# Regrouping six turned probability tiles four to two, and reordering the first steps of a tanh feed-forward, in a one-core attention and mixture kernel

## The reference, cut to what matters

```python
def _attn_ref(q, k, v, proj):                 # 2 batches, 8 heads, 768 tokens, 64 wide
    q_bucket, k_bucket = ...                  # from the signs of q @ proj, k @ proj (6 bits)
    scores = where(q_bucket[:, None] == k_bucket[None], (q @ k.T) / 8, -1e9)
    attn = exp(scores - scores.max(-1)); attn /= attn.sum(-1) + 1e-9
    return attn @ v

def _moe_ref(x, phi, w1, w2):                 # x: 1536 x 512, 32 slots, 8 experts of width 1024
    logits = x @ phi
    slot_out = experts(softmax(logits, 0).T @ x)        # 32 x 512
    return softmax(logits, 1) @ slot_out

def _moe2_ref(x, w_in, w_out):                # w_in: 512 x 2048, w_out: 2048 x 512
    h = x @ w_in
    return (h - tanh(h)) @ w_out
```

## Time and profile before

| | |
|---|---|
| median of 3 runs | 498.12 us (497.16 to 500.0) |
| the profiled execution's own time | 497.75 us |
| its span, first to last instruction | 496.0 us |
| mean granted TensorE clock | 0.990 of full |
| busy: PE, DVE, ACT, POOL | 92%, 74%, 68%, 31% |

### The profile page before, as it was taken

The page is one execution under the profiler, slowest core; times in us unless marked ns, Lnnn a source line. Parts: engine busy times, 40 slices in busy tenths (PEclk is TensorE's granted clock), DMA queues, the critical chain, the costliest instruction groups (busy, mean ns, idle before and its releaser), DMA issues.

```text
span 496.0 us, 9754 instructions
## 1 busy us (share of the span) xinstructions
PE 458.6 (92%) x3509; PEld 359.6 (73%) x3509; DVE 368.4 (74%) x779; ACT 339.1 (68%) x666; POOL 153.5 (31%) x198
## 2 busy tenths in 40 slices
PE   1599999999999999999998997987989999999996
PEld 0488888888887988979887341454767888888885
DVE  2478777877778787787886519038969999998992
ACT  3287786877868777786662126047769999999971
POOL 1044241432505325052000100004434555446530
PEclk9999999999999999999999999799999999999999
DMA  8544819357292662615609999980000020001002
GB/s 215 133 99 114 265 43 267 103 129 249 49 300 64 153 231 51 153 33 145 229 4 355 375 386 386 387 314 1 1 1 1 0 85 2 0 32 55 2 1 85
DMA packets 33840, 68.16 MB, mean 137 GB/s; under 512 B 3328, under 2 KB 5504, under 8 KB 33792
## 3 DMA queue, kind: packets, MB, share of 16 engines
q1 hardware_dynamic: 33792, 67.54, 43.5%
HBM read 58.09 MB, written 3.15 MB: 123 GB/s over the span
## 4 chain that ended last, share of the span: by engine, by line
PE 80%; DVE 8%; DMA 8%; issue 1%; SPq 1%; ACT 1%; POOL 0%; DVEq 0%; ACTq 0%
PE b L892 14%; PE b L876 13%; PE b L1054 8%; PE b L865 8%; PE b L1055 8%; PE b L1056 8%; PE b L866 7%; DMA ring_b<-in_w 3%; DMA ring_x<-in_w 3%; PE b L848 3%; PE b L979 2%; PE b L1041 2%; PE b L904 2%; DVE st L627 1%; DMA qk<-bits 1%
## 5 line engine op out<-in xcount | busy, mean ns | idle before, releaser
L627 DVE TENSOR_REDUCE st<-b 128x1 f32<-128x768 f32 x96 | 91.4, 952 | 50.8 <-PE b L866 50.7
L436 ACT ACTIVATE probs<-b,st 128x768 f32<-128x768 f32 x96 | 94.9, 988 | 35.6 <-DVE st L630 34.7
L393 POOL TENSOR_TENSOR uu<-uu,sq 128x256 f32<-128x256 f32 x94 | 74.3, 812 | 121.9 <-ACT uu L499 121.9
L876 PE MATMUL b<-const,probs 128*128 128x128 f32 x576 | 84.0, 277 | 1.0 <-DVE pt L639 0.5
L865 PE MATMUL b<-qk 96*128 96x384 f32 x192 | 75.5, 393 | 5.8 <-DMA qk<-bits 5.8
L1054 PE MATMUL b<-woh,gh 128*128 128x512 f32 x192 | 76.2, 397 | 4.5 <-DVE gl_a L765 3.4
L876 PEld LDWEIGHTS b<-const,probs 128*128 128x128 f32 x576 | 68.8, 142 | 10.1 <-DVE pt L639 5.5
L1055 PE MATMUL b<-wol,gh 128*128 128x512 f32 x192 | 75.2, 392 | 0.0
L892 PE MATMUL b<-pt,vn 128*64 128x128 f32 x1152 | 73.5, 277 | 0.7 <-ACT pt L447 0.7
L892 PEld LDWEIGHTS b<-pt,vn 128*64 128x64 f32 x1152 | 61.9, 137 | 15.1 <-ACT pt L447 9.6
L447 ACT ACTIVATE pt<-b 128x384 f32<-128x384 f32 x96 | 46.7, 487 | 32.1 <-PE b L876 32.1
(11 more groups left out here) (116 smaller groups left out, 709.1 us busy)
## 6 DMA issues: line engine op xcount, KB each, us to landing
ring<-in_w SPq DMA_DIRECT2D x15, 1024.0 KB, 8.4
ring_b<-in_w SPq DMA_DIRECT2D x12, 1024.0 KB, 11.5
raw<-in_k SPq DMA_DIRECT2D x32, 192.0 KB, 3.9
raw<-in_q SPq DMA_DIRECT2D x32, 192.0 KB, 4.3
ring_x<-in_w SPq DMA_DIRECT2D x5, 1024.0 KB, 11.3
wo_raw<-in_w_out SPq DMA_DIRECT2D x1, 4096.0 KB, 14.8
win<-in_w_in SPq DMA_DIRECT2D x4, 1024.0 KB, 14.2
vn<-in_v SPq DMA_DIRECT2D x8, 384.0 KB, 5.1
```

Of the source, the lines that this page charges most:

```text
L393: ins = pool.tensor_tensor(uu[:, r, cols], uu[:, r, cols], sq[:, r, cols], ALU.mult)
L436: act.activation(probs[:, h].rearrange("p (a n) -> p a n", a=2), score[h][:, :].rearrange("p (a n) -> p a n", a=2)[:, :, 0:HALF], ACT.Exp, ...
L627: dve.tensor_reduce(neg, score[h][:, :].rearrange("p (a n) -> p a n", a=2)[:, :, 0:HALF], AX.XY, ALU.max, negate=True).then_inc(max_done, 1)
L876: ins = pe.transpose(ptp[:, a * 512 + t * P:a * 512 + (t + 1) * P], probs[:, h, (3 * a + t) * P:(3 * a + t + 1) * P], ident[:, :])
```

## The change

It has two parts.

**In the attention**, the six turned tiles of a unit are grouped four and two instead of three and three. TensorE writes four tiles in the first bank and two in the second. ScalarE copies 512 columns where it copied 384, VectorE 256 where it copied 384. Each group is still guarded by the same semaphores.

**In the opening of the feed-forward**:

- The turned expert output goes to two banks, two products each. VectorE copies the first half, ScalarE the second; TensorE waits for both.
- On VectorE, the series and the first merge of step 0 come ahead of `first_lo(2)`, `first_lo(3)` and `copy_part(1)`; the merge waits for ScalarE's tanh of step 0 too. `copy_part(1)` comes after g of step 0.
- `low(1)` and `high(1)` move a step ahead, from step 3 to step 1 on VectorE and to step 2 on ScalarE. `split_lo(1)` moves from step 0 to step 1, behind `low(1)`.
- On ScalarE, `split_hi(1)` moves from ahead of `high(0)` in step 1 to step 2, ahead of `high(1)`; `split_hi(2)` from behind `high(2)` in step 4 to ahead of `high(3)` in step 5; `split_hi(3)` from step 8 to step 9.
- On TensorE, ten idle transposes come ahead of `fold_parts(1)` where twenty came behind it. `fold_parts(2)` moves from step 1 to step 2, and `fold_parts(3)` from step 6 to step 5.

```diff
+PT_A = 4 * P
...
-            if J == 1:
-                return 0
-            return J - LAG if J >= LAG + 1 else None
+            if J in (1, 2):
+                return J - 1
+            return J - LAG if J >= LAG + 2 else None
...
-                act.activation(pt[:, n % 2, h, 0:HALF], ptp[:, 0:HALF], ACT.Copy).then_inc(pt_a, 1)
+                act.activation(pt[:, n % 2, h, 0:PT_A], ptp[:, 0:PT_A], ACT.Copy).then_inc(pt_a, 1)
...
+            act.wait_ge(sot_done, 2)
+            act.activation(sot[:, 2:4], b01[:, 512:512 + 2 * P].rearrange("p (k s) -> p k s", k=2),
+                           ACT.Copy).then_inc(sot_ready, 1)
...
-                if J == 1:
+                if J == 2:
                     split_hi(1)
+                if J == 5:
+                    split_hi(2)
                 if lagged(J) is not None:
                     high(lagged(J))
-                if J == 4:
-                    split_hi(2)
-                if J == 8:
+                if J == 9:
                     split_hi(3)
...
-                dve.tensor_copy(pt[:, n % 2, h, HALF:S], ptp[:, 512:512 + HALF]).then_inc(pt_b, 1)
+                dve.tensor_copy(pt[:, n % 2, h, PT_A:S], ptp[:, PT_A:S]).then_inc(pt_b, 1)
...
-            dve.tensor_copy(sot[:, :, :], b01[:, 0:512].rearrange("p (k s) -> p k s", k=KT)).then_inc(sot_ready, 1)
+            dve.tensor_copy(sot[:, 0:2], b01[:, 0:2 * P].rearrange("p (k s) -> p k s", k=2)).then_inc(sot_ready, 1)
...
                     dve.wait_ge(first_series, 1)
+                    dve.wait_ge(first_tanh, 1)
...
-                if J > 1 and lagged(J) is not None:
+                if J == 0:
+                    first_lo(2)
+                    first_lo(3)
+                if J > 2 and lagged(J) is not None:
                     low(lagged(J))
...
             first_lo(0)
             first_lo(1)
-            copy_part(1)
-            first_lo(2)
-            first_lo(3)
             for J in range(STEPS):
                 tanh_and_g(J)
                 if J == 0:
+                    copy_part(1)
                     low(0)
+                if J == 1:
+                    low(1)
                     split_lo(1)
...
-                for a in range(2):
+                for a, tiles in enumerate((range(4), range(4, TILES))):
...
-            pe.wait_ge(sot_ready, 1)
+            pe.wait_ge(sot_ready, 2)
...
             hidden(2)
+            keep_warm(10)
             fold_parts(1)
-            keep_warm(20)
             hidden(3)
...
-                if J == 1:
-                    fold_parts(2)
-                if J == 6:
-                    fold_parts(3)
+                if J in (2, 5):
+                    fold_parts(2 if J == 2 else 3)
```

More of the change, by code:

```diff
@@ L207, in bucket_attention_soft_moe_tanh_ffn @@
         part_done, part_copied = sem("part_done"), sem("part_copied")
-        first_series = sem("first_series_done")
+        first_series, first_tanh = sem("first_series_done"), sem("first_tanh_done")
         wp_done, wst_hi, wst_lo = sem("slots_in_done"), sem("wst_hi"), sem("wst_lo")
@@ L500, in elementwise @@
                 if J == 0:
-                    act.activation(th[:, r], h, ACT.Tanh)
+                    act.activation(th[:, r], h, ACT.Tanh).then_inc(first_tanh, 1)
                 act.activation(mk[:, r], sq[:, r], ACT.Relu, scale=1.0, bias=small[:, 255:256]).then_inc(mk_done, 1)
@@ L871, in turn_probs @@
                 pe.wait_ge(exp_done, u + 1)
-                for a in range(2):
+                for a, tiles in enumerate((range(4), range(4, TILES))):
                     if u:
                         pe.wait_ge((pt_a, pt_b)[a], u)
-                    for t in range(3):
-                        ins = pe.transpose(ptp[:, a * 512 + t * P:a * 512 + (t + 1) * P],
-                                           probs[:, h, (3 * a + t) * P:(3 * a + t + 1) * P], ident[:, :])
+                    for t in tiles:
+                        ins = pe.transpose(ptp[:, t * P:(t + 1) * P], probs[:, h, t * P:(t + 1) * P], ident[:, :])
                     ins.then_inc(pt_written, 1)
@@ L1025, in _ @@
             for kt in range(KT):
-                ins = pe.matmul(b01[:, kt * P:(kt + 1) * P], so[:, kt * P:(kt + 1) * P], foldr[:, :].bitcast(F32),
-                                start=True, stop=True)
-            ins.then_inc(sot_done, 1)
+                ins = pe.matmul(b01[:, kt // 2 * 512 + kt % 2 * P:kt // 2 * 512 + (kt % 2 + 1) * P],
+                                so[:, kt * P:(kt + 1) * P], foldr[:, :].bitcast(F32), start=True, stop=True)
+                if kt % 2:
+                    ins.then_inc(sot_done, 1)
             hb = (b01[:, 0:512], b01[:, 512:1024], b23[:, 0:512], b23[:, 512:1024])
```

## The result

The changed kernel takes 485.99 us (median of 4 runs, 485.69 to 486.79) against 497.78 us (4 runs) of the kernel before: a ratio of 0.9758, 95% interval 0.9725 to 0.9791, 11.8 us faster. Forecast were 489.6 us and a range of 486.5 to 493.0.

A forecast was written before the change was run, and what follows sets the result against it. TensorE's own time and small gaps were taken to bound the attention, VectorE the feed-forward's opening. Gains of 2.6 and 5.9 us (7.3 - 1.4) took 497.75 to 489.2; the median's 0.37 made it 489.6, range 486.5 to 493.0.

The forecast's parts named there:

- The removed wait's own term: Attention: 28 weight loads no longer wait for VectorE's copy, 0.14 us each, 3.9 us gained.
- The term for ScalarE's copy: Attention: ScalarE's longer copy makes the next unit's first load late, charged 0.05 us 28 times; bounds 0 and 0.14 each.
- The end of the stage: End of the attention: VectorE's last copy, 0.13 us shorter, stands alone ahead of the last `weigh`; 0.1 us gained.
- The walk through the opening: Feed-forward's opening: queues lined up by durations; `products(0)` 3.4, `products(1)` 4.5 and `products(8)` 7.3 us earlier.
- the 0.9 us of slack: Opening, steps 2 to 8: VectorE needs 19.2 us and keeps up with TensorE by under a microsecond.
- The walk's last step: From `products(8)` on: TensorE is always busy, so every microsecond gained at its start comes off the end.
- The clock: Opening, around `products(1)`: the granted clock falls again, some 2.1 us lost, 0.7 absorbed ahead of `products(2)`; charged 1.4 us, bounds 0 and 3.
- the early cases: Nothing lost to the clock, or ScalarE's attention copy in time: 1.4 us more each, 486.8 to 488.2 us; chance 0.20.
- ScalarE taking VectorE's place: Attention: the first load waits 0.14 us for ScalarE's copy, so nothing is gained there, 492.2 us; chance 0.13.
- VectorE failing to keep up by 3 us: Opening up to step 8: VectorE becomes the bound, `products(7)` and `products(8)` wait 3 us as before, 492.6 us; chance 0.10.
- half the clock for 13 us: Opening, steps 1 to 4 at half clock: its gain is gone, half the attention's stays, 497 us; chance 0.05.
- the slower case: Attention: ScalarE becomes the bound in steps preparing the next pair; 504 us at 0.3 us a pair; chance 0.05.

The follow-up runs named there:

- e2: The changed kernel with the attention's old grouping of three tiles and three, so the opening's part alone: 490.80 us.
- e6: The changed kernel with ScalarE's attention copy of 512 columns made in four instructions of 128: 490.96 us.
- e7: The changed kernel with the turned expert output in one bank and one VectorE copy of 512 columns, as before: 485.95 us.
- e4: The changed kernel with `hidden(5)` behind `products(1)` instead of ahead of it: 485.94 us.
- e5: The changed kernel with the attention's groups turned round, two tiles copied by ScalarE and four by VectorE: 503.49 us.
- e12: The changed kernel with `hidden(5)` behind `products(1)`, `copy_part(2)` and `copy_part(3)` on ScalarE, and GpSimd's series in four instructions of 128 columns, not two of 256: 486.51 us.

## Why the prediction was right and wrong

**The mechanism of the attention** was right: the removed wait, the sizes of both copies, their starts. Its gain was put at 2.6 us and measured 4.75. The removed wait's own term, 28 x 0.14 = 3.9 us, is what 29 pairs of 0.135 give. *The term for ScalarE's copy*, 28 x 0.05 = 1.4 us, is the step that failed: the loader waits 0.09 us and the matmuls don't. I had named zero as a bound for just that reason and taken a value towards the late end. *The end of the stage* was 0.1 us in the sum; the three single intervals, two of them at the end, gave some 0.8, which the waits' view had not shown. One reading was off without harm: the spacing of the loads in the earlier trace rows is (0.42 - 0.14) / 2 = 0.14 us and not 0.12, which leaves VectorE's shorter copy more room.

**The walk through the opening** was right in its order and nearly in its size. Distances from `first_columns` as forecast (335.6, 342.85, 347.55 and 367.7 less 326.63) and as measured in the changed kernel and, without a fall of the clock, in e2: `products(0)` 8.97, 9.08, 9.09; `products(1)` 16.22, 16.27, 16.22; `products(8)` 41.1, 41.72, 41.91. `products(2)`, forecast after 20.92 us, came after 20.48 in e2, so the loss lies between it and `products(8)`. VectorE didn't have the 0.9 us of slack there that the walk gave it: in e2, e6 and e7 `products(8)` waits 0.68 us for `low`, which I had named as a sign of being wrong. I had shared its access with GpSimd in the walk and then tested VectorE's sum with the steady rate, while in e4 the predicated copies took 1.26 to 1.30 us in five of eight steps. The walk's last step, that all that is gained at `products(8)` comes off the end, was also too much: 6.3 us there are 5.8 at `products(47)`.

**The clock** was the other failed step. The fall came where forecast and somewhat shorter (3.2 us at 1.2 GHz, where 2.1 us lost mean 4.2). Its price at `products(8)` was not 1.4 us but nothing: that starts after 41.72 and 41.64 us in the two executions with the fall (changed, e5) and after 41.91, 41.88 and 41.89 in the three at full clock (e2, e6, e7). Up to `products(7)` the loss is there (38.55 against 37.90 in e2). It then falls into the 0.68 us for which TensorE waits ahead of `products(8)` for VectorE in e2, and in the changed kernel doesn't. I had compared the loss with the wait ahead of `products(2)` alone and not with those further on. By `products(47)` the executions with the fall are 0.3 us behind the others (156.44 and 156.35 against 156.09 to 156.12), which is the price in the end.

**What was luck.** The opening gave 6.3 + 0.31 = 6.65 us by `products(8)` and 5.8 + 0.31 = 6.1 us by `products(47)`, forecast 5.9. That this is close is chance: the clock's charge of 1.4 us was 1.1 too high, and the walk's 7.3 us about as much too hopeful. So nearly all of what the sum missed by the distances, 10.9 us measured against 8.5, is the attention's.

**The rivals.** Of the early cases ScalarE's copy in time is what happened whole, the clock at nearly no price too; they had a chance of 0.20 and times of 486.8 to 488.2. ScalarE taking VectorE's place, VectorE failing to keep up by 3 us, half the clock for 13 us and the slower case didn't occur. e5 reached the slower one's time, 503.49 us, but by VectorE's copy; e6 shows that ScalarE's would be felt at once if it were longer. What is between 10.9 us and the 12.1 us of the two profiled executions is the start's 1.67 us (first weighted products at 28.89 and 27.22) less 0.4 us by which the changed execution was longer in the weights' stage, the 0.31 of e7 counted; both stretches differ that much between executions. 10.9 us off 498.12 would be 487.2, inside the range. 10.9 also lies within the interval of the ratio, 10.4 to 13.7 us. So as far as the distances go, the median's place below the range, and not in its lower end, is how the executions happened to fall.

## What to carry to other kernels

A wait on the weight loader is not yet one of the matmuls: read the distance between matmuls, or the period of the loop, ahead of charging it, and count gains by periods as well as by waits. Time lost on an engine costs only what is left when the next wait of that engine on another has swallowed it, so carry a loss through to the last such wait, and a gain to the end of the kernel: here 0.5 of 6.3 us were lost again. In a pipeline that starts up, a copy or fold asked for by an in-order queue one step too early or too late costs the whole chain: here two such places cost 3.4 us each when either was taken back, and the grouping of six tiles by how late each copying engine stands was worth 4.7.

## What the runs showed that was not expected

A loop's period tells differences that no time here could: plain pairs took 4.64, 4.50, 4.67 and 4.88 us in the four variants, each repeated within some 0.02 us. The landing of the first transfers moved the start of the attention by 2.5 us between executions (26.8 to 29.3 us), as much as most of the differences looked for here. And GpSimd's multiplication of 128 columns takes 0.59 us where 256 take 0.85, so each of the 94 instructions that e12 halved cost GpSimd 0.28 us more (26 us in all).
